# A fused attention, expert and gated layer on one core: branches per absent tile, ACT tables and third tile moved, odd mixes and stores reordered

## The reference, cut to what matters

```python
kv  = einsum('bhsd,bhse->bhde', k, v)                # 8 x 8 heads, 576 x 64
o   = einsum('bhsd,bhde->bhse', q, kv)
x   = o / sqrt(mean(o*o) + 1e-6) * g_norm            # -> x [4608, 512]
logits = x @ w_gate + modality_bias[modality_id]     # 8 experts
e   = argmax(logits);  p = softmax(logits)[e]
y[token] = p * (relu(x[token] @ w1[e]) @ w2[e])      # 512 -> 1024 -> 512
out = (sigmoid(y @ W_gate) * (y @ W_val)) @ W_out    # 512 -> 1536 -> 512
```

## Time and profile before

| | us |
|---|---|
| median of 3 runs (1472.45, 1479.63, 1479.74) | 1479.63 |
| the profiled execution, and its span | 1477.0, 1475.2 |
| PE busy | 1378.5 (93%) |
| DVE, ACT, POOL busy | 902.8 (61%), 444.2 (30%), 295.6 (20%) |

### The profile page before, as it was taken

One profiled execution on the slowest core, in us unless ns is written; L12 is line 12 of the kernel. 1 busy time (PEld: TensorE's weight loads), 2 busy tenths in 40 slices (PEclk: granted clock), 3 DMA queues, 4 the chain that ended last, 5 costly groups with the idle time before them and its releaser, 6 DMA issues.

```text
span 1475.2 us, 25202 instructions
## 1 busy us (share of the span) xinstructions
PE 1378.5 (93%) x8290; PEld 1134.3 (77%) x8291; DVE 902.8 (61%) x1525; ACT 444.2 (30%) x768; POOL 295.6 (20%) x354
## 2 busy tenths in 40 slices
PE   4767789999999999798899999999999999999997
PEld 4656578878888888677778888888888888888886
DVE  3667877787577864456665557555565556655551
ACT  3665222222222222334332224222242222322231
POOL 0054445434444443112010001100011000010011
PEclk9877899999999999999999999999999999999999
DMA  9983366777567756479965442654417444044420
GB/s 345 345 313 122 98 182 197 221 208 213 155 189 211 218 165 145 124 248 364 283 209 177 150 150 79 177 178 151 151 57 207 176 149 156 22 179 150 150 78 30
DMA packets 132435, 262.70 MB, mean 178 GB/s; under 512 B 20200, under 2 KB 85736, under 8 KB 126208
## 3 DMA queue, kind: packets, MB, share of 16 engines
q1 hardware_dynamic: 73216, 200.33, 41.0%
q10 hardware_dynamic: 47936, 31.58, 8.5%
q0 software_dynamic: 11200, 29.69, 6.1%
HBM read 179.44 MB, written 51.73 MB: 157 GB/s over the span
## 4 chain that ended last, share of the span: by engine, by line
PE 79%; DVE 6%; DMA 6%; issue 4%; ACT 2%; SPq 1%; DVEq 1%; ACTq 0%; POOL 0%; POOLq 0%
PE ps L1695 31%; PE ps L1675 17%; PE ps L1537 13%; PE ps L1523 12%; DMA mixes<-mix 3%; PE ps L1554 1%; PE ps L1503 1%; PE ps L1665 1%; DMA vt<-in_v 1%; PE ps L1579 1%; PE ps L1707 1%; DMA hq<-h 1%; SPq L575 0%; DVE mix L1366 0%; DVE ew L1025 0%
## 5 line engine op out<-in xcount | busy, mean ns | idle before, releaser
L1695 PE MATMUL ps<-a_hi,st 128*128 128x512 f32 x1344 | 421.4, 389 | 0.9 <-DVE u L1443 0.9
L1695 PEld LDWEIGHTS ps<-a_hi,st 128*128 128x128 f32 x1344 | 252.4, 188 | 54.0 <-DVE a_lo L1401 1.5
L1675 PE MATMUL ps<-wo,shi 128*128 128x512 f32 x816 | 255.4, 394 | 9.1 <-DVE slo L1410 8.2
L1695 PE MATMUL ps<-a_lo,st 128*128 128x512 f32 x672 | 261.4, 389 | 0.0
L1537 PE MATMUL ps<-ew,hhi 128*128 (+1 forms) x640 | 201.4, 396 | 13.1 <-DVE hlo L1213 13.1
L1523 PE MATMUL ps<-ew,xhi 128*128 (+1 forms) x640 | 199.5, 393 | 1.9 <-DVE xlo L1131 1.9
L1675 PEld LDWEIGHTS ps<-wo,shi 128*128 128x128 f32 x816 | 154.3, 190 | 45.6 <-issue 5.3
L724 POOL DMA_INDIRECT out<-ot,out_tok x36 | 35.5, 986 | 718.2 <-ACT ot L892 712.7
L1675 PE MATMUL ps<-wo,slo 128*128 128x512 f32 x408 | 161.7, 396 | 0.0
L1537 PEld LDWEIGHTS ps<-ew,hhi 128*128 128x128 f32 x640 | 122.5, 192 | 40.8 <-issue 15.1
L1695 PEld LDWEIGHTS ps<-a_lo,st 128*128 128x128 f32 x672 | 126.1, 188 | 26.2
(11 more groups left out here) (242 smaller groups left out, 1834.2 us busy)
## 6 DMA issues: line engine op xcount, KB each, us to landing
st<-mixes SPq DMA_DIRECT2D x48, 1792.0 KB, 7.2
raw<-in_moe_w SPq DMA_DIRECT2D x64, 512.0 KB, 5.0
hq<-h ACTq DMA_DIRECT2D x160, 128.0 KB
mixes<-mix SPq DMA_DIRECT2D x24, 512.0 KB, 8.3
kt<-in_k SPq DMA_DIRECT2D x8, 1152.0 KB, 9.4
vt<-in_v SPq DMA_DIRECT2D x8, 1152.0 KB, 12.0
qt<-in_q SPq DMA_DIRECT2D x8, 1152.0 KB, 7.6
xg<-xs ACTq DMA_DIRECT2D x144, 64.0 KB
```

Source lines behind the costliest of these rows:

```text
L1675: last = mm(ps[:, 4 + m, :], s[:, rows], wo[f // 2][:, w, f % 2], start=(f == 0 and w == 0 and s is shi[slot]), stop=(f == GC - 1 and s is ...
L1695: last = mm(bank_of(f, idx), st[f % 2][:, at:at + 128], x[:, idx, k, :], start=(k == 0 and w == 0 and x is a_hi), stop=(k == 1 and w == 1))
```

## The change

On every engine the body of the unrolled list for a tile above `FULL` (for POOL: from its second extra step on) gets one If around it, inside which the old Ifs stay. SP loads only half of tile 2, ACT the other half. On ACT Exp moves ahead of `hhi_of` of tile 0, Sigmoid's table is asked for there instead of behind the tiles, and the second half of `h` of tile 1 moves ahead of `xhi` of tile 2. On DVE the gate values move behind the turning of tile 2, `pad_rows` behind `hlo` of tile 1, `compact_rows` behind the turning of tile 3. In the first block `mixes_of` of odd pieces moves from the end of f = 1, 4, 7 to behind `slo` of f = 2, 5, 8. SP stores pieces 4 and 5 in another order, and its one wait for all stores is cut up over the loads of `st`; DVE waits for the last `mix` stores before the first `s1`, which lies over `mix`. `load_first` waits for one tile more per buffer.

```diff
@@ -383,7 +383,7 @@
...
         t13_made, t24_made, thi_made, tlo_made = (sem(n) for n in ("t13_made", "t24_made", "thi_made", "tlo_made"))
-        b_out, b_out_late, t_out = sem("b_out"), sem("b_out_late"), [sem(f"t_out{n}") for n in range(4)]
+        b_out, b_out_late, t_out = sem("b_out"), [sem(f"b_out_late{n}") for n in range(2)], [sem(f"t_out{n}") for n in range(4)]
         st_in = [sem(f"st_in{n}") for n in range(2)]
...
@@ -440,13 +440,17 @@
...
 
-        def tiles(engine, step, after={}):
+        def tiles(engine, count, step, after={}):
 
...
             for n in range(FULL - 2, NT + 1):
-                step(0, n, True)
+                if n <= FULL:
+                    step(0, n, True)
+                else:
+                    with engine.If(count > n - 1):
+                        step(0, n, True)
                 if n in after:
...
@@ -534,7 +538,7 @@
...
             sp.wait_ge(xt_made, SOON)
-            load_quarters(sp, Tile(0, SOON), (0, 1, 2, 3))
+            load_quarters(sp, Tile(0, SOON), (2, 3))
             sp.wait_ge(gates_made, 1)
...
@@ -566,7 +570,7 @@
...
                     dst = mixes[2 * n:2 * n + 2, :, 768 * w:768 * w + 768].rearrange("f p x -> p f x")
-                    sp.dma_start(dst, src).then_inc(b_out if n < 4 else b_out_late, 16)
+                    sp.dma_start(dst, src).then_inc(b_out if n < 4 else b_out_late[n - 4], 16)
 
...
@@ -591,24 +595,31 @@
...
             for n in range(PIECES):
-                store_plain(n)
+                if n < 4:
+                    store_plain(n)
                 if n + 2 < PIECES:
...
                     load_wo(n + 1)
-                if n + 2 >= PIECES:
+                if n == 5:
                     mixed(n)
...
                 store_mixes(n)
+                if n == 4:
+                    load_y(0, n - 4)
+                if n >= 4:
+                    store_plain(n)
             sp.wait_ge(b_out, 16 * 8)
-            sp.wait_ge(b_out_late, 16 * 4)
-            for op in range(4):
-                sp.wait_ge(t_out[op], 16 * PIECES)
             for n in range(SUPERS * GC):
...
                     sp.wait_ge(pe_p, 7 * (n - 1))
+                if n < 2:
+                    sp.wait_ge(b_out_late[n], 16 * 2)
+                if n < GC and n % 2 == 0:
+                    for op in range(4):
+                        sp.wait_ge(t_out[op], 16 * (n // 2 + 1))
                 sp.dma_start(st[n % 2][:].bitcast(F32), mixes[n % GC]).then_inc(st_in[n % 2], 16)
...
@@ -706,7 +717,11 @@
...
             for n in range(FULL - 2, NT + 2):
-                tile_step(0, n)
+                if n <= FULL + 1:
+                    tile_step(0, n)
+                else:
+                    with pool.If(use.count > n - 2):
+                        tile_step(0, n)
 
...
@@ -798,7 +813,7 @@
...
                 for p in range(2):
-                    act.wait_ge(y_out[p], 16 * ((BLK // 128 + E) // 2))
+                    act.wait_ge(y_out[p], 16 * ((BLK // 128 + E + SOON) // 2))
                 for g in range(4):
...
@@ -848,16 +863,18 @@
...
             h_of(Tile(0, 0), 1)
-            hhi_of(Tile(0, 0))
             act.wait_ge(exp_asked, 1)
             nc.scalar.activation(r_ex[:], r_d[:], ACT.Exp).then_inc(exp_made, 1)
+            nc.scalar.activation(tiny[:, 1:2], ident[:, 0:1], ACT.Sigmoid)
+            hhi_of(Tile(0, 0))
             h_of(Tile(0, 1), 0)
+            load_x(Tile(0, 2), (0, 1))
+            h_of(Tile(0, 1), 1)
             xhi_of(Tile(0, 2))
-            h_of(Tile(0, 1), 1)
             hhi_of(Tile(0, 1))
...
             use = Use(act)
-            tiles(act, tile_step, {FULL - 1: load_first, FULL + 2: y_high})
+            tiles(act, use.count, tile_step, {FULL - 1: load_first, FULL + 2: y_high})
 
...
@@ -952,7 +969,6 @@
...
 
-            nc.scalar.activation(tiny[:, 1:2], ident[:, 0:1], ACT.Sigmoid)
             high(0)
...
@@ -1319,17 +1335,17 @@
...
             nc.vector.memset(y[:, :, D:YW], 0.0)
+            x_turned(Tile(0, 2))
             gate_values()
-            x_turned(Tile(0, 2))
             xlo_of(Tile(0, 2))
             h_turned(Tile(0, 1))
+            hlo_of(Tile(0, 1))
             pad_rows()
-            hlo_of(Tile(0, 1))
+            x_turned(Tile(0, 3))
             compact_rows()
-            x_turned(Tile(0, 3))
             use = Use(dve)
             y_of(Tile(0, 0))
-            tiles(dve, tile_step, {FULL + 1: y_turned, FULL + 3: y_low})
+            tiles(dve, use.count, tile_step, {FULL + 1: y_turned, FULL + 3: y_low})
 
...
@@ -1419,8 +1435,8 @@
...
                         low_out(f // 3 * 2 + 1)
+                    if f % 3 == 2 and f < 9:
                         mixes_of(f // 3 * 2 + 1)
-                    if f % 3 == 2 and f < 9:
                         low_mix(f // 3 * 2 + 1)
...
@@ -1461,6 +1477,9 @@
...
                     dve.wait_ge(sig1_made, n + 1)
+                    if isinstance(i, int) and i == 0 and f == 0:
+                        for op in range(4):
+                            dve.wait_ge(t_out[op], 16 * PIECES)
                     nc.vector.tensor_tensor(s1_of(f), c22[:], u3[:], ALU.mult).then_inc(s1_made, 1)
...
@@ -1652,7 +1671,7 @@
...
             pe.wait_ge(tok_step, 1)
-            tiles(pe, tile_step)
+            tiles(pe, use.count, tile_step)
 
...
```

## The result

| | before | after |
|---|---|---|
| median, 9 runs each on one chip | 1477.05 us | 1470.7 us |
| lowest and highest | 1472.45, 1480.81 | 1467.96, 1475.05 |
| profiled execution | 1477.0 us | 1470.21 us |
| its span | 1475.2 us | 1468.4 us |

The ratio is 0.996 [0.9941, 0.9978]: 5.9 us, with 3.2 to 8.7 in the interval. A second batch (12 runs of it) gave 0.9954 [0.9937, 0.997].

A forecast was written before the change was run, and what follows sets the result against it. TensorE was taken as the bound wherever it isn't kept waiting. Gains of 4.7 (start), 1.3 (entry) and 7.7 (first block), together 13.7 us, come off the profiled 1477.0 us: 1463.3, kept as 1463, range 1456 to 1473.

The forecast's parts named there:

- Start: Start of the experts: hidden table loads, third tile's split loads and DVE's new order gain 4.7 us, bounds 2 to 6.
- 0 to 1 is lost here, and I take 0: Start, DVE's `y_of`: later gate values delay the gates' gather, costing 0 to 1 us, priced at 0.
- Entry: Between last tile and first block: fewer branches for absent tiles bring the first gate product 1.3 us sooner, bounds 0 to 2.9.
- Rival E: Entry: each absent tile's jump must fetch code, gain gone from 3.1 us each; 1487 us at 5 each; chance 0.04.
- First block: First block: odd mixes behind the next `s` cut the loss from 12.7 to 5.0 us, gain 7.7, bounds 3 to 11.
- the mixes of piece 4 end at 697.9: First block: earlier stores of pieces 1 and 3 let piece 4's mixes end at 697.9 us, 699.7 before.
- 14 us later: Block's end: TensorE wants the first `st` load at 731.7, 14 us behind its issue at about 717.6; nothing gained or lost.
- each us beyond would count in full: Block's end: if the queue ate all the `st` load's 14 us cover, each further us would add fully to the time.
- Rival A: First block: DMA engines set the pieces' pace, waits move to even pieces; block 4, entry 1, total 1467 us; chance 0.17.
- B: First block: freer queue gives 13.3 us per piece, all 11 us return, entry gives 2.5; total 1459 us; chance 0.13.
- C: Behind the branches Sigmoid's table is loaded again, 1.3 us on the path; start gives only 2; total 1467 us; chance 0.05.
- D: Little gain: start 2, block 3 less two slow starts of 1.8, entry 0; total 1474 us; chance 0.11.

The follow-up runs named there:

- `st` first: The changed kernel with the first load of `st` issued ahead of piece 5's stores; median 1472.87 us, ratio 0.9953 to the kernel before.

## Why the prediction was wrong, point by point

**Start, 4.7 forecast, 3.6 measured** (37.0 in the three profiles without this part, 33.4 in the mean of 14 with it). The tables are hidden as forecast, three loads in all. The prediction weighed a page of the Trainium skill (ScalarE: Activation LUTs, What ACT_TABLE_LOAD costs), which has a drain beside each load: the rows show each load 1.28 us long and its activation 1.30 behind the load's start, and the cast of `hhi` 0.15 us behind `ht`. The trace was right. TensorE's wait at the first half of tile 1 went away as forecast. What fails is the line "0 to 1 is lost here, and I take 0", and its reason: DVE waits 1.0 us ahead of `y_of`, but not for the gates. The transpose of tile 3 that I counted as merely moved had covered that time. It is most of the 1.1 us missing: `xlo` of tile 3 starts 24.9 us behind the first product with `xhi` of tile 1, where the forecast has 23.8 and before 28.3.

**Entry, 1.3 forecast.** The direction is right, and the count of branches was a poor price. ACT's walk fell by 1.7 us with no table load behind it, DVE's by only 1.2, where 19 branches less at 0.112 would be 2.1. TensorE's gap went from 2.94 to 1.28 us, near the forecast, but it lies between 1.28 and 3.2 in kernels with the same Ifs (2.4 in the mean of 16, 2.6 in that of three without). In seven of the 16 it ends with a wait for DVE's `wo`, in two of the three with one for `gv`. And 1.07 of the 1.66 us were lost again just ahead of the gap, since the last 24 products of tile 39 took 8.59 us for 7.52, more of them at the lower clock (last section). The whole stage is 9.87 in after, 10.17 in the mean of 16 profiles with the Ifs, and 10.29 in that of three without: a gain of 0.1 to 0.6. The branches alone give 0.9988 [0.9971, 1.0004]. Rival E, a fetch at each jump that costs over 3.1 us, is excluded: no gap was longer than 3.2 in all.

**First block, 7.7 forecast, 2.2 measured (1.6 by the means below).** This is the step that failed: that the ring of mixes would run faster, so that the waits taken from the odd pieces would not come back at the even ones. The forecast had "the mixes of piece 4 end at 697.9", 57.9 us behind the first output product at 640.0. They end at 697.01, which looks right only because the block starts 3.7 us earlier: it is 60.7 behind 636.28, against 59.7 before. Up to piece 4 the ring got no faster from stores issued 0.8 us sooner; with 0.8 MB less in each turn it did, by 2.3 us. Piece 5 did come sooner, 13.3 us behind piece 4 for 16.3, and the wait at output 8 went with it as forecast; but that is behind output 7, where the loss is. I had this pace in the rows (14.3 per piece) and called it the buffer's, with the engines' work in it; then I let it shrink. From it follows:

- output 7 starts 66.1 us behind output 0, where unhindered it would be 58.7: 7.4 lost for 3.7 forecast. Waits of 0.55, 1.60, 0.56 and 3.84 make 6.55, and slow products behind them the rest.
- the output step behind the wait of 3.84 takes 4.44 us for 2.80 (702.42 to 706.86): 1.65 more. I had counted slow steps behind the old waits, but none behind the new one.
- the first `st` load was issued at 719.02, 82.7 us behind output 0, where the forecast has 77.6 (717.6 less 640.0). It lands in 14.3 us behind the last stores and is 1.29 late. The "14 us later" was just what the queue ate, and "each us beyond would count in full" was too much: with `st` first TensorE is idle for 1.35 us at the same place, for DVE's `s`, the 1.3 that the prediction had put there.

That is 3.1 lost at the end where 1.3 were forecast, and 10.5 where 5.0 were in all.

**Rivals.** Rival A describes what happened up to output 7: "the waits only move from the odd pieces to the even ones". Its argument, the share of 0.95, isn't the evidence, since 0.81 with the same pace and 0.98 with no waits for `slo` both occur. Its 4 us for the block were still too many. B is excluded, C too (no table is loaded again). D's sum, 1474, is as near to the median of 1470.7 as A's 1467. One reading of the rows was too wide: waits for `hlo` and `slo` are "by far the most" only behind the attention; over the whole trace TensorE waits 13.1 and 8.2 us for them, and 13.1 for `vt` in the attention.

**Sum.** 3.6 for the start, 0.1 to 0.6 for the entry, 1.55 or nothing for the clock behind it, and 1.6 for the block (mean of four profiles with the new block 96.9, of three with the old 98.5): 5.3 to 7.4, against 5.9 timed. The prediction had no term for the clock, so whatever it gave is luck.

## What to carry to other kernels

When a wait sits behind a buffer ring, measure the ring's pace over several turns first, and find the bytes or the work that lie in its loop. If the edit takes none of them out, price it as moving the wait to the next reader, and look for the one with the least slack. An instruction moved out of a place may have covered a delay there that no row of before shows. And a DMA share near 1 says little on its own: ask which transfers are between one use of the buffer and the next.

## What the runs showed of the hardware

The 48 gate products ahead of the block (two steps) come at two speeds. The windows from the first product with `hhi` of tile 39 to the first gate product, and from there to the first output product, before:

```profile
616.70:627.10 10.40, 7.52 (x24) 5.74 (x24) 6.82 (x14) 4.42 (x5) 2.40 (x1) 0.82 0.09 32
627.20:640.00 12.80, 12.80 (x49) 10.25 (x50) 4.67 (x6) 4.16 (x6) 3.63 (x3) 0.87 0.55 135
```

and after:

```profile
615.20:625.00 9.80, 8.56 (x24) 6.47 (x24) 6.79 (x14) 3.04 (x3) 2.40 (x1) 0.69 0.10 34
625.00:636.30 11.30, 11.26 (x49) 9.17 (x50) 4.93 (x6) 4.16 (x6) 4.11 (x3) 1.00 0.62 153
```

The same products take 12.79 us at a mean granted clock of 0.87 and 11.24 at 1.00, which is 2.4 GHz throughout. Shorter windows show where the clock was at 0.50, which is 1.2 GHz. Before:

```profile
613.70:620.50 6.80, 3.80 (x9) 3.03 (x10) 5.79 (x11) 2.44 (x3) 1.85 (x1) 0.50 0.01 2
627.40:630.70 3.30, 3.30 (x9) 2.51 (x9) 0.61 (x1) 0.00 (x0) 2.65 (x3) 0.50 0.12 43
```

and after:

```profile
614.60:621.30 6.70, 6.13 (x14) 4.79 (x15) 4.36 (x10) 2.04 (x3) 2.40 (x1) 0.50 0.13 46
```

In both kernels TensorE is idle for 5.2 us ahead of the last tile's products, and the clock is at 0.50 in their first part: for 3.8 us of the products before, for 6.1 in after. Only before has a second slow stretch, right behind its gap of 2.94 us; after, with a gap of 1.28, has none (its clock is 1.00 from 621.4 to 636.3). Over all kernels the 11.24 goes with a gap ahead of the first gate product of 2.12 us or less (six kernels), 12.6 to 12.8 with one of 2.37 or more (thirteen). So the shorter gaps went with 1.55 us more. I hadn't priced this, and what decides it is open, since the gap itself varies with the same code.

Queued behind 1.5 MB of loads, each of a piece's four stores (2.1 MB together) lands 8.5 us behind its issue in the median; ahead of the loads 4.4; on POOL's queue beside them 9.9. In these runs the order in the queue decided who was late, and fewer bytes (128 KB for 512 KB in each `graw` load) brought the stores' landing from 8.5 to 6.7. Whether a correct kernel can take loads out of that stretch (`graw` or `wraw` earlier, into room that is free by then) wasn't tried and is what these runs point to. The kernel with small `graw` loads computes other numbers and rests on two runs and one profile. Against after its ratio of 0.9894 is worth 9 to 10 us more, which is an estimate of the size, not a forecast for a correct kernel.
